# A mixture-of-experts tail with its eight experts written out, the next rows turned in banks of their own, and their copies moved to GpSimd

## The reference, cut to what matters

```python
do_compute = x @ w_skip > 0
xc = x[do_compute]
logits = xc @ w_gate                      # [tokens, 8]
e_idx = np.argmax(logits, axis=1)
gate_w = softmax(logits)[e_idx]
for e in range(8):                        # w1[e]: 384 x 1024, w2[e]: 1024 x 384
    h = np.maximum(xc[e_idx == e] @ w1[e], 0.0)
    y[e_idx == e] = gate_w * (h @ w2[e])
out = x.copy(); out[do_compute] = xc + y
```

## Time and profile before

| | us |
|---|---|
| median of 3 runs (lowest, highest) | 828.02 (826.68, 828.31) |
| the profiled execution's own time | 827.14 |
| its span, first to last instruction | 825.4 |
| PE busy in the span | 784.1 (95%) |
| DVE, ACT, POOL busy | 568.2, 370.4, 112.2 |

### The profile page before, as it was taken

The page is one execution under the profiler, slowest core; times in us unless marked ns, Lnnn a source line. Parts: engine busy times, 40 slices in busy tenths (PEclk is TensorE's granted clock), DMA queues, the critical chain, the costliest instruction groups (busy, mean ns, idle before and its releaser), DMA issues.

```text
span 825.4 us, 29106 instructions
## 1 busy us (share of the span) xinstructions
PE 784.1 (95%) x12083; PEld 714.3 (87%) x12084; DVE 568.2 (69%) x1504; ACT 370.4 (45%) x1042; POOL 112.2 (14%) x281
## 2 busy tenths in 40 slices
PE   6977999999999999999999999999999989999993
PEld 3546888999999998999999999999999989999993
DVE  6979888778677786777778686645323657767751
ACT  3733533534344343454425444353533466666641
POOL 1000000001020100101002010100103044344441
PEclk9998999999999999999999999999999999999997
DMA  8772021222311313022221211111124646656510
GB/s 280 221 234 66 27 73 48 85 67 66 98 41 48 91 54 104 22 67 82 83 66 41 72 41 57 56 41 47 40 78 129 192 142 204 196 182 192 184 32 15
DMA packets 48089, 79.75 MB, mean 97 GB/s; under 512 B 5840, under 2 KB 35498, under 8 KB 47968
## 3 DMA queue, kind: packets, MB, share of 16 engines
q1 hardware_dynamic: 44544, 73.07, 27.4%
q0 software_dynamic: 3424, 4.93, 1.9%
HBM read 67.05 MB, written 13.19 MB: 97 GB/s over the span
## 4 chain that ended last, share of the span: by engine, by line
issue 78%; POOL 9%; DMA 6%; PE 3%; POOLq 2%; DVE 1%; SPq 1%; ACT 0%
DMA id_table<-token,slot 5%; POOL idle L695 3%; POOL kq_t L750 2%; POOL id_table L740 2%; PE psum L995 2%; POOL ids_all L746 1%; DMA id_table<-x_sb 1%; POOL out L805 1%; DMA x_sb<-kq 1%; POOLq L521 0%; PE psum L851 0%; POOLq L522 0%; PE psum L996 0%; POOLq L772 0%; SPq L575 0%
## 5 line engine op out<-in xcount | busy, mean ns | idle before, releaser
L1029 PE MATMUL psum<-xt_hi,w_hi 128*128 128x256 f32 x768 | 226.2, 295 | 5.9 <-issue 2.7
L1030 PE MATMUL psum<-xt_lo,w_hi 128*128 128x256 f32 x768 | 217.5, 283 | 0.0
L1031 PE MATMUL psum<-xt_hi,w_lo 128*128 128x256 f32 x768 | 217.3, 283 | 0.0
L1205 ACT ACTIVATE h_raw<-psum 128x256 f32<-128x256 f32 x192 | 73.9, 385 | 318.2 <-PE psum L1031 316.5
L1465 DVE TENSOR_TENSOR h_lo<-h_raw,h_hi 128x256 fp32r<-128x256 f32 x192 | 81.4, 424 | 155.7 <-ACT h_hi L1206 146.5
L1029 PEld LDWEIGHTS psum<-xt_hi,w_hi 128*128 128x128 f32 x768 | 145.3, 189 | 15.5 <-issue 8.8
L1031 PEld LDWEIGHTS psum<-xt_hi,w_lo 128*128 128x128 f32 x768 | 146.3, 191 | 0.0
L1030 PEld LDWEIGHTS psum<-xt_lo,w_hi 128*128 128x128 f32 x768 | 145.8, 190 | 0.0
L1053 PE MATMUL psum<-w_hi,h_hi 128*128 128x394 f32 x384 | 138.3, 360 | 0.8 <-DVE h_lo L1465 0.8
L1055 PE MATMUL psum<-w_hi,h_lo 128*128 128x394 f32 x384 | 131.1, 341 | 0.0
L1054 PE MATMUL psum<-w_lo,h_hi 128*128 128x394 f32 x384 | 131.0, 341 | 0.0
(11 more groups left out here) (189 smaller groups left out, 1103.1 us busy)
## 6 DMA issues: line engine op xcount, KB each, us to landing
kq_t<-kq SPq DMA_DIRECT2D x24, 512.0 KB, 3.5
bp<-moe_w SPq DMA_DIRECT2D x24, 512.0 KB, 5.3
kv_t<-kv SPq DMA_DIRECT2D x24, 384.0 KB, 3.1
bp<-moe_w SPq DMA_DIRECT2D x24, 384.0 KB, 4.9
kd<-kq SPq DMA_DIRECT2D x20, 256.0 KB
x_table<-x_sb SPq DMA_DIRECT2D x13, 392.0 KB, 3.1
out<-x_sb SPq DMA_DIRECT2D x12, 384.0 KB
bp<-moe_w_in SPq DMA_DIRECT2D x6, 512.0 KB, 6.3
```

The costliest lines, as they stand in the source:

```text
L1029: m(out, hi, x_hi, start=first, stop=False)
L1030: m(out, hi, x_lo, start=False, stop=False)
L1031: return m(out, lo, x_hi, start=False, stop=last)
L1205: a_.activation(h_raw[i % 2][:, :], up_ps[i % 2][:, 0:G2], ACT.Silu)
```

## The change

- `expert_bounds` and the pair loop go. `experts` is written out for eight experts. Each reads one bound, its last tile, and takes the last of the expert before as its first. On SP the six loads of weights are written out too, and the addresses are constants.
- `turn_ps` is new: the transposes write banks 6 and 7. Both halves are turned in round 8, ahead of the wait for h_lo. ACT and DVE read them there.
- POOL copies xg_in to xg at the head of its tile, behind a hold for y of the tile before and one for the gathered rows. ACT no longer does. The largest logit moves from round 3 to 5 on DVE, the exponentials from round 4 to 6 on ACT.
- ACT runs a relu on `primer` behind the schedule, ahead of its first copies of xt_hi.
- DVE signals plan_ready once `ends` is there, forms xt_lo of tile 0, and then computes `starts`, signalled as starts_ready. POOL gathers the rows of tile 0 ahead of loading the ids of tile 1.

```diff
+        turn_ps = [psum[:, 6 + g, 0:KD * C] for g in range(2)]
...
-        def expert_bounds(eng, e):
-            first = eng.value_load(ends[0:1, bass.ds(e, 1)], min_val=0, max_val=MAXT)
-            last = eng.value_load(ends[0:1, bass.ds(e + 1, 1)], min_val=1, max_val=MAXT)
-            return first, last
...
             eng.wait_ge(plan_ready, 1)
-            with eng.Fori(0, E // 2 - 1) as pair:
-                for i in range(2):
-                    one(pair * 2 + i, i, True)
-            for i in range(2):
-                one(E - 2 + i, i, i == 0)
+            first = 0
+            for e in range(E):
+                last = eng.value_load(ends[0:1, e + 1:e + 2], min_val=1, max_val=MAXT)
+                one(e, e % 2, e < E - 1, first, last)
+                first = last
...
-            with sp.Fori(0, E // 2 - 1) as pair:
-                for i in range(2):
-                    last = sp.value_load(ends[0:1, bass.ds(pair * 2 + i + 1, 1)], min_val=1, max_val=MAXT)
-                    expert_weights(pair * 2 + i + 2, i, last * EN)
+            for e in range(E - 2):
+                last = sp.value_load(ends[0:1, e + 1:e + 2], min_val=1, max_val=MAXT)
+                expert_weights(e + 2, e % 2, last * EN)
...
             load_ids(0, ids_next, first_in)
-            pool.wait_ge(plan_ready, 1)
-            load_ids_of(1)
             pool.wait_ge(table_stored, 16 * NP)
             pool.wait_ge(out_stored, 16 * NP)
             hold(xgt_ps[1], 1)
             hold(first_in, 32).then_inc(ids_free, 1)
             gather_rows(ids_next, xg_gathered)
+            pool.wait_ge(starts_ready, 1)
+            load_ids_of(1)
             hold(xg_gathered, 32)
...
+                with pool.Fori(first, last_t) as t:
+                    hold(y_ready, t + 1)
+                    hold(xg_gathered, t * 32 + 32)
+                    for a in range(2):
+                        last = g.tensor_copy(xg[a], xg_in[a])
+                    last.then_inc(xg_copied, 1)
                     hold(xg_copied, t + 1)
...
             def transposes(t, a):
                 pe.wait_ge(xg_gathered, t * 32 + 32)
                 for x in range(KD):
-                    last = tr(up_ps[a][:, C * x:C * x + C], xg_in[a][:, C * x:C * x + C], ident[:, :])
+                    last = tr(turn_ps[a][:, C * x:C * x + C], xg_in[a][:, C * x:C * x + C], ident[:, :])
...
+                        if n == M2:
+                            for a in range(2):
+                                transposes(t + 1, a)
                         if n >= 2:
                             d = n - 2
                             pe.wait_ge(eh_lo_ready, t * M2 + d + 1)
                             if d == 0:
                                 pe.wait_ge(y_ready, t + 1)
-                            if n >= M2:
-                                transposes(t + 1, n - M2)
...
+            act.wait_ge(y_ready, 1)
+            a_.activation(primer[:, 2:3], primer[:, 1:2], ACT.Relu)
...
-                        if n == 2:
-                            act.wait_ge(y_ready, t + 1)
-                            act.wait_ge(xg_gathered, t * 32 + 32)
-                            for a in range(2):
-                                last = cp(xg[a], xg_in[a])
-                            last.then_inc(xg_copied, 1)
-                        if n == 4:
+                        if n == 6:
                             act.wait_ge(gate_top, t + 1)
...
-            d.tensor_copy(ends, ends_f)
+            d.tensor_copy(ends, ends_f).then_inc(plan_ready, 1)
+            for b in range(2):
+                dve.wait_ge(xgt_hi[b], 1)
...
-            d.tensor_scalar(starts, starts_f, float(E * N - G2), None, ALU.min).then_inc(plan_ready, 1)
+            d.tensor_scalar(starts, starts_f, float(E * N - G2), None, ALU.min).then_inc(starts_ready, 1)
...
-                        if x == 3:
+                        if x == 5:
                             dve.wait_ge(xg_copied, t + 1)
```

More of the change, by code:

```diff
@@ L119, in program @@
         minus = h_hi[:, 0, 0:P]
-        primer = sb("primer", [1, 2])
+        primer = sb("primer", [1, 3])
         pairs = sb("pairs", [P, 4, 2])
@@ L264, in program @@
         out_stored, table_stored = sem("out_stored"), sem("table_stored")
-        plan_step, plan_ready = sem("plan_step"), sem("plan_ready")
+        plan_step, plan_ready, starts_ready = map(sem, ("plan_step", "plan_ready", "starts_ready"))
         ids_loaded, xg_gathered, xg_copied, ids_copied = map(sem, ("ids_loaded", "xg_gathered", "xg_copied", "ids_copied"))
@@ L655, in expert_weights @@
                         sp.wait_ge(ew_split, split + n + 1)
-                    src, width, _ = piece_of((w1[bass.ds(e, 1)].rearrange("e a b -> (e a) b"),
-                                              w2[bass.ds(e, 1)].rearrange("e a b -> (e a) b")), (i, i), n, EPIECES, FE, W2_AT)
+                    src, width, _ = piece_of((w1[e:e + 1].rearrange("e a b -> (e a) b"),
+                                              w2[e:e + 1].rearrange("e a b -> (e a) b")), (i, i), n, EPIECES, FE, W2_AT)
                     dst = e_stage[n][:, 0:width]
@@ L781, in _, with one @@
             gather_rows(ids_next, xg_gathered)
+            pool.wait_ge(starts_ready, 1)
+            load_ids_of(1)
             hold(xg_gathered, 32)
-            def one(e, i, more):
-                first, last = expert_bounds(pool, e)
-                with pool.Fori(first, last) as t:
+            def one(e, i, more, first, last_t):
+                with pool.Fori(first, last_t) as t:
[4 more added lines that the diff above has]
+                    last.then_inc(xg_copied, 1)
                     hold(xg_copied, t + 1)
@@ L1106, in transposes, with one @@
                 for x in range(KD):
-                    last = tr(up_ps[a][:, C * x:C * x + C], xg_in[a][:, C * x:C * x + C], ident[:, :])
+                    last = tr(turn_ps[a][:, C * x:C * x + C], xg_in[a][:, C * x:C * x + C], ident[:, :])
                 last.then_inc(xgt_ps[a], 1)
-            def one(e, i, more):
-                first, last_t = expert_bounds(pe, e)
+            def one(e, i, more, first, last_t):
                 with pe.Fori(first, last_t) as t:
@@ L1252, in xt_parts, with one @@
                     act.wait_ge(xgt_ps[a], t + 1)
-                    cp(xt_hi[0][:, :, C * a:C * a + C], up_ps[a][:, 0:KD * C].rearrange("p (k c) -> p k c", k=KD)).then_inc(xgt_hi[a], 1)
-            def one(e, i, more):
-                first, last_t = expert_bounds(act, e)
+                    cp(xt_hi[0][:, :, C * a:C * a + C], turn_ps[a].rearrange("p (k c) -> p k c", k=KD)).then_inc(xgt_hi[a], 1)
+            def one(e, i, more, first, last_t):
                 with act.Fori(first, last_t) as t:
@@ L1570, in _ @@
             then(d.tensor_reduce(ends_f, part, AX.X, ALU.add))
-            d.tensor_copy(ends, ends_f)
+            d.tensor_copy(ends, ends_f).then_inc(plan_ready, 1)
+            for b in range(2):
+                dve.wait_ge(xgt_hi[b], 1)
+                d.tensor_tensor(xt_lo[0][:, FIRST[b]:FIRST[b + 1], :], first_ps[:, FIRST[b]:FIRST[b + 1], :],
+                                f32(xt_hi[0][:, FIRST[b]:FIRST[b + 1], :]), ALU.subtract).then_inc(xgt_lo[b], 1)
             then(d.tensor_scalar(jump, tiles_f[:, 0:E - 1], -float(G2), float(N), ALU.mult, ALU.add))
@@ L1578, in _ @@
             then(d.scalar_tensor_tensor(starts_f, tile_no[0:1, :], float(G2), starts_f, ALU.mult, ALU.add))
-            d.tensor_scalar(starts, starts_f, float(E * N - G2), None, ALU.min).then_inc(plan_ready, 1)
-            for b in range(2):
-                dve.wait_ge(xgt_hi[b], 1)
-                d.tensor_tensor(xt_lo[0][:, FIRST[b]:FIRST[b + 1], :], first_ps[:, FIRST[b]:FIRST[b + 1], :],
-                                f32(xt_hi[0][:, FIRST[b]:FIRST[b + 1], :]), ALU.subtract).then_inc(xgt_lo[b], 1)
+            d.tensor_scalar(starts, starts_f, float(E * N - G2), None, ALU.min).then_inc(starts_ready, 1)
             def xt_parts(t):
@@ L1587, in xt_parts, with one @@
                     dve.wait_ge(xgt_hi[a], t + 1)
-                    d.tensor_tensor(xt_lo[0][:, :, C * a:C * a + C], up_ps[a][:, 0:KD * C].rearrange("p (k c) -> p k c", k=KD),
+                    d.tensor_tensor(xt_lo[0][:, :, C * a:C * a + C], turn_ps[a].rearrange("p (k c) -> p k c", k=KD),
                                     f32(xt_hi[0][:, :, C * a:C * a + C]), ALU.subtract).then_inc(xgt_lo[a], 1)
-            def one(e, i, more):
-                first, last_t = expert_bounds(dve, e)
+            def one(e, i, more, first, last_t):
                 with dve.Fori(first, last_t) as t:
```

## The result

The change makes the kernel slower: 832.79 us median (828.16 to 837.47, 20 runs) against 826.52 (823.09 to 828.31, 20 runs) for the kernel before on the same chip. The ratio is 1.0078, 95% interval 1.0062 to 1.0093. The forecast was 824.8, reckoned from the 828.02 of three runs; against the 826.52 measured beside it, the change was to save 3.2, and it costs 6.3.

A forecast was written before the change was run, and what follows sets the result against it. The prediction took PE, busy 95% of the span, as the bound. Savings of 0.9 (tile 0), 1.6 (tiles 1 to 5), 0.6 (tile 6) and 0.1 (tile 7), together 3.2, took 828.02 to 824.8 us; range 820.0 to 829.0.

The forecast's parts named there:

- Base and banks: Expert tiles on PE: floor 17.65; own banks and both transposes at once save 0.32 a tile, giving 17.7 with table ahead.
- The 0.32 for the head: Tile head on PE: the 0.37 wait for xt_lo goes, 0.05 is left for h_lo.
- in waits that stay: Register loads per expert on ACT, DVE and POOL: removing one was counted as nothing.
- Table ahead: ACT's table reloads at experts 2 and 4 go, loaded behind the last x2 instead; two tiles get back 0.61.
- Handoff: Start of the experts: signal 1.5 earlier, PE starts at 662.6 to 663.1 instead of 664.36, gaining 1.3 to 1.7.
- the first gathers themselves hang on DMAs that don't move: Tile 0's gathers stay in time, so tile 1's rows come at 679.7 to 680.9 and tile 0 gains only 0.9.
- A clock fall would be hidden by the same wait: Tile 0: a clock fall behind the handoff, priced 1.35, would be covered by PE's wait for tile 1's rows.
- POOL's copies: POOL between scatter and gather: copies 0.5 each, one to two splits in the way, stall 0.5, period 18.2.
- the forecast's own slack: Gathers on POOL, now starting 5.79 after y, may start 0.46 later before PE stalls.
- rival C: POOL between scatter and gather: copies lose to splits every tile, gathers from 7.2 after y, 831.2 at most; chance 0.14.
- The bad end of the sum: Whole kernel: tile 0 loses 0.9, tiles 1 to 5 lose 2.9, the end gains 0.6, giving 831.2.
- DVE behind POOL: Splits against POOL's copies: by the skill's rule splits are held up 0.5 per copy, covered by DVE's idle time; no row showed it.

The follow-up runs named there:

- e1: Changed kernel with the copies of the gathered rows back on ACT: 824.20 us, ratio 0.9977 to the kernel before.
- e8: Changed kernel with the row copies back on ACT and the handoff signal of before: 823.68 us, ratio 0.9950 to the kernel before.
- e6: Changed kernel with rows gathered a tile ahead; behind y POOL copies, gathers, then scatters: 826.74 us, ratio 1.0003 to the kernel before.
- e14: Changed kernel in e6's order, POOL's loop ending a tile sooner with the last scatter alone behind it: 819.40 us, ratio 0.9906 to the kernel before.
- e9: Kernel before with only own banks for the turned rows and both halves turned in round 8: 825.06 us, ratio 0.9975.
- e11: Kernel before with only the experts written out, one bound each, and the Relu ahead: 824.81 us, ratio 0.9980.
- e15: e14 with the handoff of the kernel before, starts formed ahead of the signal: 818.12 us, ratio 0.9890 to the kernel before.
- e4: Kernel before with only the gathered rows copied by POOL (logit and exponentials in rounds 5 and 6): 830.21 us, ratio 1.0060.
- e3: Changed kernel, but SyncE waits for the landed first rows before loading expert 2's weights: 830.23 us, ratio 1.0055 to the kernel before.
- e12: Changed kernel with the handoff of before, same source as e2 run again: 828.45 us, ratio 1.0003 to the kernel before.
- e2: Changed kernel with the handoff of before, signal behind the starts: 828.46 us, ratio 1.0010 to the kernel before.
- e10: Changed kernel, rows gathered a tile ahead, copied twice through a third buffer, scatter first behind y: 825.34 us, ratio 0.9979 to the kernel before.

## Why the prediction was wrong

**Base and banks: right together.** The forecast had 17.7 for a tile that waits for nothing; e1, e8, e6 and e14 show 17.8. The 0.32 for the head was costed apart from the register loads, which were put at nothing "in waits that stay". What goes with them does matter once xt_lo is off the path (0.62 against 0.23 behind y, e9 and e8). The change has both parts, so the sum did not suffer.

**Table ahead: right in size, not in place.** Two tiles were to get back 0.61 each; e11 shows 1.28 for both. But the Relu put ahead loads no table. It runs in 0.18 at 652.53, and the one load stands at the first loop's head:

```profile
652.53 0.18 ACT L1249 ACTIVATE primer<-primer 1x1 f32<-1x1 f32 x1
...
659.44 1.28 ACT L1263 ACT_TABLE_LOAD   x1 [0.50 <-issue]
```

Writing the experts out is what removed the reloads: e11 has this one load in the experts, and its Relu ahead loads nothing either. The load that stayed is followed by the 0.40 for h_lo in tile 0, which e15 with its later start doesn't have.

**Handoff: right at its start, wrong in what it sets off.** PE's first matmul came 1.70 sooner, where 1.3 to 1.7 was forecast. e11 gives 0.96 of it to the writing out; the signal itself is 0.7 to 0.9. The clock stayed up, but that isn't shown to be the work of the shorter wait: behind waits of 2.75 (e4) and 2.78 (e9), with the handoff of before, it stayed up as well. The step that failed is "the first gathers themselves hang on DMAs that don't move". They met DMAs that came to move towards them: the weight loads are released by splits, and so by PE's start. The early signal and the writing out brought them from 12.3 to 9.6 after the mark, beside the first gather, and the splits beside its issue. The first rows landed at 16.2, where the forecast had POOL ready at 12.7 (670.77). The second part of the miss is POOL behind it: 3.75 from those rows to the next gather, where before it was 2.76 and the forecast's holds give some 2.2 to 3.4. The forecast took 1.68 of that for a wait on ACT. It is POOL's own queue: e4, which waits for no engine there, has the same 1.68 (0.86 when written out).

```profile
671.72 0.33 POOL L695 TENSOR_TENSOR idle<-half 1x1 f32<-1x1 f32 x2 [1.68 <-issue]
```

Together the rows of tile 1 were there at 27.2 in place of 22.2, outside the forecast of 679.7 to 680.9 (21.6 to 22.8). In order of time, 3.7 of the 5.0 are there before any copy is made. But the parts don't simply add: with the copies back on ACT (e1) the first gather is as late, and the rows come 3.1 sooner all the same. e3 undoes the collision with the weights and gets back 1.7 in tile 0; e12 keeps the old signal and gets back 4.7 there. Why the ids of tile 0 landed later, and why runs of e2 and e12 spread over 13 us, stays open.

**"A clock fall would be hidden by the same wait": right for the fall it meant, blind to another.** The forecast saw a fall behind the handoff, whose cost the rows' wait would cover. e4 and e9 had none and still took 19.95 and 19.84 for tile 0, waiting 1.48 and 1.73 for rows. The fall that mattered came in the rows' wait, where nothing covers it, and cost about 2.

**POOL's copies: the start right, the landing wrong.** Forecast: 0.5 a copy, one split in the way, the gather starting 6.2 after y. Measured: 0.48, one split, 6.06, in all of tiles 1 to 6. By the forecast's own slack (5.79 + 0.46) PE should never have waited; it waited in all five tiles, a few tenths in tiles 1 and 2 and 0.80 to 1.23 in the next three. The term that was missing is the gather's issue itself. It is held up by the splits too, and takes 1.92 in tiles 1 to 6, in place of 1.07; in tile 7, which has no splits, it takes 1.07. The trace of before had it already in tile 0, with 1.62 beside a split; the forecast read only the 1.07 of tile 3. In the group of all gathers of rows the mean went from 1096 ns to 1374, after and before here:

```profile
L746 POOL DMA_INDIRECT kq_t<-x_table,ids_all x20 | 27.5, 1374 | 5.7 <-issue 5.7
```

```profile
L750 POOL DMA_INDIRECT kq_t<-x_table,ids_all x20 | 21.9, 1096 | 6.1 <-issue 6.1
```

From issue to landing it was 7.1; now it is 7.7 to 8.9, of which 0.85 are the issue. Up to 0.9 more pass in tiles 3 to 5, in the stretch that the gather shares with the weight loads; in tile 6, where no weights are loaded, it was 4.4 before and is 5.3 now, the issue's part alone. So rows land 13.8 to 14.9 after y, where 13.34 was the limit. The forecast took 18.2 a tile; they took 18.69 (93.43 / 5), and a saving of 1.6 became a loss of 0.8. That is rival C's place and nearly its price, though not by its rule: it was to decide from gathers 7.2 after y, and they were at 6.06.

**Sum.** Tiles 1 to 5 miss the forecast by 2.4 and tile 0, with its start, by 6.7: it was to gain 0.9 and lost 5.8. The second is the larger error. The bad end of the sum, 831.2, held for the profiled execution (830.03) and not for the median. It allowed tile 0 a loss of no more than 0.9, because the bound was made from one more split, and not from a first gather that comes late itself.

**Copies against splits.** The Trainium skill ("SBUF — State Buffer", Who interferes with whom) says that a VectorE instruction with two SBUF inputs and a GpSimd one that reads SBUF exclude each other, whichever came first. The trace agrees for the copies and the splits. DVE behind POOL was open in the forecast; it is shown by the 1.93 at 710.00 and by the group of 24 splits of 128x1024, 1224 ns on average before and 1398 after. The 1.21 of e10 is another case, as that operation has one input in SBUF. DVE's idle time covered the longer splits in the changed kernel, as forecast; e10's gate operation stood where no idle time covered it.

## What to carry to other kernels

An earlier start moves all that hangs on it. List the transfers that are released by the engine that starts sooner, and ask which small transfer, on whose landing a wait hangs, they will now run beside; here PE started 1.7 sooner and ended the first tile 5.8 later. Slack in front of a gather has to be counted up to its landing, with the issue priced beside the work that will then run. And where a buffer is on a long chain (copy, gather, turn), another order a tile ahead (e14, e15: 8 to 9 us under the kernel before) was worth more than any choice of engine for the copy (e8: 4), as long as nothing of it is left behind the last tile. A price is best read in the stage that it is for: the slow issue stood in tile 0 of the old trace, and the forecast used tile 3.

## What the runs showed of the hardware

- An indirect gather's issue on POOL took 1.0 to 1.1 beside idle or small work of DVE and 1.92 where a two-input split of 128x1024 ran at its start: the issue is held up too, not only POOL's arithmetic.
- A copy of 128x392 floats took 0.48 to 0.50 on POOL, and the pair 0.96 even where a split waited for it.
- A gate operation of 128x2 on DVE took 1.21 until POOL's copies were done (e10), against 0.16 on average in the changed kernel.
- The first gather, alone, was seen landed 2.05 after its second issue ended (670.59 - 668.54) and 2.09 in e3; beside weight loads 4.0 (671.17 - 667.16).
- The clock was at 1.2 GHz behind waits of PE of 6.78 (after), 2.74 (before) and 1.90 (e12, at the handoff). It stayed at 2.4 GHz behind 2.92 (e12, before the transposes), 2.78 (e9) and 2.75 (e4, both at the handoff), 1.73 (e15) and 1.02 (after). So the length of the last wait alone doesn't say which. A window of e12 behind the handoff:

```profile
664.00:665.00 1.00, 1.00 (x6) 1.00 (x6) 0.38 (x1) 0.39 (x1) 0.13 (x1) 0.50 0.03 1
```
